# Twenty unread products before the first mask, and the second batch's keys turned two heads later

## The reference

```python
# attention: 2 batches, 8 heads, 576 rows, 64 columns a head
scores = q @ k.T / sqrt(64)
mask = scores >= (32nd largest score of the row)
attn = softmax(where(mask, scores, -1e9))
x = (attn @ v), heads side by side           # 1152 x 512
# mixture of 8 experts, all of them dense, F = 1024
P = exp(x @ w_gate - max), 8 rounds of row and column normalisation
x = sum over e of P[:, e] * (relu(x @ w1[e]) @ w2[e])
# last block, F = 2048
h = x @ w_in;  g = h * tanh(softplus(h));  out = g @ w_out
```

## Time and profile before

| | us |
|---|---|
| median of 3 executions | 1240.41 (1239.22 to 1242.2) |
| the profiled execution | 1242.88 |
| its span, first to last instruction | 1241.0 |
| PE busy | 1198.6 (97%) |
| DVE busy | 899.6 (72%) |
| ACT busy | 687.6 (55%) |
| POOL busy | 642.6 (52%) |

### The profile page before, as it was taken

One profiled execution on the slowest core, in us unless ns is written; L12 is line 12 of the kernel. 1 busy time (PEld: TensorE's weight loads), 2 busy tenths in 40 slices (PEclk: granted clock), 3 DMA queues, 4 the chain that ended last, 5 costly groups with the idle time before them and its releaser, 6 DMA issues.

```text
span 1241.0 us, 19573 instructions
## 1 busy us (share of the span) xinstructions
PE 1198.6 (97%) x6676; PEld 1071.3 (86%) x6676; DVE 899.6 (72%) x1556; ACT 687.6 (55%) x1226; POOL 642.6 (52%) x393
## 2 busy tenths in 40 slices
PE   4878999999999999999999999999999999999998
PEld 4777889999999998999888999999888888898777
DVE  6989998899999971446646564646464647887886
ACT  5666776767777664442243333333333337888776
POOL 1857965555656567763376666666666630000000
PEclk8599999999999999999999999999999999999999
DMA  9023432233323233332233222222222122222230
GB/s 170 9 86 120 144 104 93 94 94 107 110 90 111 86 111 102 120 102 93 85 106 107 69 75 76 75 80 74 86 67 94 52 68 85 69 69 84 86 125 36
DMA packets 150486, 112.10 MB, mean 90 GB/s; under 512 B 34832, under 2 KB 124944, under 8 KB 150416
## 3 DMA queue, kind: packets, MB, share of 16 engines
q1 hardware_dynamic: 150416, 111.19, 29.6%
HBM read 104.09 MB, written 7.08 MB: 90 GB/s over the span
## 4 chain that ended last, share of the span: by engine, by line
PE 86%; DVE 7%; ACT 3%; POOL 2%; issue 2%; DMA 1%; SPq 0%; ACTq 0%; DVEq 0%; POOLq 0%
PE ps L903 16%; PE ps L728 15%; PE ps L741 15%; PE ps L964 14%; PE ps L1031 7%; PE ps L1087 7%; PE ps L637 4%; PE ps L608 3%; DVE top L1486 2%; DVE work L1488 2%; PE ps L618 2%; PE ps L597 1%; POOL s_sb L1961 1%; PE ps L632 1%; POOL e_sb L1964 1%
## 5 line engine op out<-in xcount | busy, mean ns | idle before, releaser
L1890 POOL TENSOR_TENSOR w_lo<-w_raw,w_hi 128x1024 fp32r<-128x1024 f32 x90 | 219.6, 2440 | 114.4 <-ACT w_hi L1114 114.3
L1114 ACT ACTIVATE w_hi<-w_raw 128x1024 fp32r<-128x1024 f32 (+1 forms) x172 | 179.4, 1044 | 0.6 <-DMA w_raw<-in_k 0.6
L1486 DVE MAX8 top<-work 128x8 f32<-128x576 f32 x216 | 152.3, 747 | 0.0
L728 PE MATMUL ps<-x_hi,w_hi 128*128 128x384 f32 (+3 forms) x384 | 128.2, 334 | 0.1
L728 PE MATMUL ps<-x_hi,w_lo 128*128 128x384 f32 (+3 forms) x384 | 127.4, 332 | 0.0
L728 PE MATMUL ps<-x_lo,w_hi 128*128 128x384 f32 (+3 forms) x384 | 127.2, 331 | 0.0
L1897 POOL TENSOR_TENSOR ha_lo<-h_f,ha_hi 128x384 fp32r<-128x384 f32 (+1 forms) x72 | 72.0, 999 | 90.4 <-ACT ha_hi L1191 90.4
L903 PE MATMUL ps<-w_hi,h_lo 128*128 128x512 f32 x296 | 117.1, 396 | 0.0
L903 PE MATMUL ps<-w_lo,h_hi 128*128 128x512 f32 x296 | 116.9, 395 | 0.0
L903 PE MATMUL ps<-w_hi,h_hi 128*128 128x512 f32 x296 | 115.3, 390 | 0.0
L1488 DVE MATCH_REPLACE8 work<-top,work 128x576 f32<-128x576 f32 x144 | 105.9, 743 | 0.0
(11 more groups left out here) (185 smaller groups left out, 3273.1 us busy)
## 6 DMA issues: line engine op xcount, KB each, us to landing
w_raw<-in_moe_w SPq DMA_DIRECT2D x288, 256.0 KB, 3.0
w_raw<-in_moe_w_in SPq DMA_DIRECT2D x32, 256.0 KB, 2.8
w_raw<-in_moe_w_out SPq DMA_DIRECT2D x32, 256.0 KB, 3.1
spill<-y_out SPq DMA_DIRECT2D x5, 768.0 KB, 3.8
y_in<-spill SPq DMA_DIRECT2D x5, 768.0 KB, 4.4
q_parts<-in_q SPq DMA_DIRECT2D x18, 128.0 KB, 3.3
vones<-in_v SPq DMA_DIRECT2D x8, 256.0 KB, 4.9
out<-acc SPq DMA_DIRECT2D x8, 256.0 KB, 2.7
```

The lines of the kernel that those rows point to most:

```text
L728: last = nc.tensor.matmul(ps[:, bank, 0:w], wt[:, s, 0, c * P:(c + 1) * P], xt[:, c, token:token + w], start=(n == 0), stop=(n == len(term ...
L1114: return nc.scalar.activation(dst, src, ACT.Copy)
L1486: last = v_.max(top[:, b, op // 2, :], src)
L1890: g_.tensor_tensor(w_lo[:, s, :, :].rearrange("p a n -> p (a n)"), w_raw[:, s, :, :].rearrange("p a n -> p (a n)"), w_hi[:, s, :, :].rearr ...
```

## The change

TensorE's and ScalarE's programs of a tile turn and copy chunk `c` of the second batch's keys at the end of head `c + 3` instead of head `c + 1`: heads 3 to 7 of tile 1 instead of 1 to 5. Both waits inside are the same ones, counted from `c`. And TensorE issues twenty products of 128 x 512 into bank 7 (`X_BANK`), which nothing reads, in head 4 of tile 0: behind the waits for the queries' and keys' copies, ahead of the wait for the first mask.

```diff
+        KEYS_AT = 3
@@ TensorE, tile_body
                     if first and h == 4:
                         pe.wait_ge(q_copied, 4)
                         pe.wait_ge(k_copied, KEYS_0)
+                        keep_clock()
                     if late_parts is not None:
                         probs_transposed(late, (h - 4) % H)
...
-                    if keys and 1 <= h <= KC:
-                        pe.wait_ge(k_high, KC + h)
-                        pe.wait_ge(k_low1, h)
-                        if h == 1:
+                    if keys and KEYS_AT <= h < KEYS_AT + KC:
+                        c = h - KEYS_AT
+                        pe.wait_ge(k_high, KC + c + 1)
+                        pe.wait_ge(k_low1, c + 1)
+                        if c == 0:
                             pe.wait_ge(q_copied, 4)
                         else:
-                            pe.wait_ge(k_copied, KEYS_0 + 2 * h - 2)
-                        keys_transposed(1, h - 1, 0)
-                        keys_transposed(1, h - 1, 1)
+                            pe.wait_ge(k_copied, KEYS_0 + 2 * c)
+                        keys_transposed(1, c, 0)
+                        keys_transposed(1, c, 1)
+
+            def keep_clock():
+
+                for _ in range(20):
+                    nc.tensor.matmul(ps[:, X_BANK, :], q_s[:, 0, 0, :], k_s[:, 0, 0, 0:4 * P], start=True, stop=True)
@@ ScalarE, tile_body
-                    if keys and 1 <= h <= KC:
-                        keys_copied(1, h - 1, 0)
-                        keys_copied(1, h - 1, 1)
+                    if keys and KEYS_AT <= h < KEYS_AT + KC:
+                        keys_copied(1, h - KEYS_AT, 0)
+                        keys_copied(1, h - KEYS_AT, 1)
```

## The result

The change makes the kernel slower: median 1242.51 us (1238.91 to 1244.72, 18 executions) against 1240.51 us before (1239.22 to 1242.8, 18 executions), ratio 1.0015 with a 95% interval of 1.0008 to 1.0022. The forecast was 1238.1 us with a range up to 1241.5. A second series of the same kernel gave 1242.56 us against 1239.9 for the kernel before, ratio 1.0021 (1.0012 to 1.0030).

What follows compares the result with a forecast made beforehand. TensorE bounds the kernel from 130.7 us; ahead of it VectorE's search is the long string, with 4.64 us of stalls. Terms 2.2 + 0.5 - 0.6 = 2.1, taken as 2.3: 1240.41 - 2.3 = 1238.1 us, range 1235.4 to 1241.5.

Steps and rivals of the forecast that it cites:

- Part 1: Tile 1, heads 1 and 2: without key transposes, tile 0's row sums start 2.2 (high clock, 60%) or 0.6 us earlier.
- The sum: Gains and costs at 130 us: 2.2 + 0.5 - 0.6 = 2.1 us at high clock, 0.5 at low; 2.3 taken.
- both ends: Tile 0's last value products: clock high, gain 2.2 us (certain if transposes do not count as busy), or low, 0.6.
- Part 2: Tile 0, head 4: twenty products hold the clock up, making head 4 faster; +0.5 us taken, between -0.6 and +0.8.
- The case in between: Tile 0, head 4: clock falls at 26.7 us, twenty products end at 31.5, 1.4 late; later places about 0.6 later.
- rival (c): Tile 0: at low clock the twenty products hold TensorE until 33.8 us, delaying POOL's masks; slower, 1243.4 us; chance 8%.
- Part 3: Tile 1, heads 6 and 7: arriving keys delay scores (1,7) or the row sums; cost 0 to 1.4 us, 0.6 taken.
- The handing on to the end: From DVE's stall to 130 us: a DVE shift at 71 us reaches the end, except for the moved keys' cost.
- Rival (b): Tile 0's last value products run at low clock without the key transposes; gain 0.7 us, 1239.7 us; chance 22%.

## Why the prediction was wrong

**Part 1, the keys leave heads 1 and 2: this step failed.** Its sum was read from one execution in which TensorE was the late one, at the low clock from 47.3 to 64.2 us, so that 1.71 us of key transposes stood on the chain. In the second trace of before TensorE stands idle 1.50 and 1.12 us around the same transposes, they cost nothing, and the stall at the row sums is 0.30 instead of 3.81 us: what part 1 wanted to take out was not there. Measured, the term that was put at a gain of 2.2 or 0.6 us is a loss of 2.3 us (1.0021 twice). I named the other side of it, that the unbroken run which lets the clock rise gets shorter, and gave it 40% and a price of 1.6 us less gain; it was priced as a smaller gain where it is a loss. What the runs show in its place is both a rise that fails to come (two traces) and, which part 1 did not have, a fall of a clock that was up, in the longer waits (three traces). Whether the step holds in executions that go like the one I read stays open: the moved keys with six products at tile 2, in a trace whose clock was low as there until 43.6 us, had a span of 1238.6 against 1241.0, but the unmoved keys with the same six, in a trace as much alike, had 1238.4. I took one profiled execution, 2.5 us above the median of its kernel, as the place to work out a gain of 2 us.

**The sum.** Its own cases give 2.1 us with the clock high for the last value products and 0.5 with it low; at 60% for the first that is 1.5 us, 1238.9. I wrote 2.3, above the better of the two cases, for a reason (the profiled execution had the favourable case) that argues for less. That is an error of the sum beside that of the mechanism; without it the forecast would still have been a gain.

**The rule on transposes.** The Trainium skill says of the transpose mode, under "TensorE: Matmul & The Clock Gate", Part 4, that it does not count as busy for the clock in the same way as products do. The trace lists the transposes here as MATMUL with the identity and does not show whether they run in that mode. For these 32-bit ones the measurement decides, and it says that they do count: sixteen of them, unread, are the only difference between a kernel whose clock is low from 63.4 to 73.4 us and one in which it is up from 49.6 to 83.2, and between ratios of 1.0021 and 1.0001. I had kept both ends open; the trace's was right, and it was the end that speaks against the change.

**Part 2, the twenty products.** The case in between came true in both traces of the change: the clock fell at 26.3 and 26.4, the products took 6.4 us and ended at 32.3 and 31.8, against 31.5 worked out; they began at 26.1 and 25.6 instead of 25.3. After them the clock stayed high until 36.5, then fell before the first value products, as forecast. The term taken was +0.5 us, near the bound for products that run mostly at the high clock, where the case in between had been worked out at -0.6. Measured, the products alone are 0.5 us slower (0.04%, not told from nothing), so that the term was about 1 us too high, inside its bounds; rival (c) has the mechanism right (forty products: 4.0 to 4.7 us later) and the size wrong for twenty.

**Part 3, the keys arrive in heads 6 and 7.** Taken as 0.6 us. The traces of the change show neither a wait for the scores of (1,7) nor a longer one at tile 1's row sums (0.53 us, as before). With fuller heads the clock no longer fell at about 84 us: it does in all seven traces with unmoved keys (once from 75 to 85) and in one of the twelve with moved ones. With keys in place and sixteen transposes more, one trace has a wait of 0.70 us for (1,7) and the ratio is 1.0005; the moved keys with unread transposes have one of 0.32 us in their second trace. The term cannot be told from 0 nor from the 0.6 us that was taken.

**The handing on to the end.** That a shift of DVE at 71 us arrives at the end held in part: TensorE's wait for mask (2,3) at 128 us was not in my list, and in five of nine traces of kernels with moved keys and no products there the clock fell right behind it, for 3.4 us, which cost 1.2. Of the five such traces with unmoved keys one has it. Whether that share is due to the keys or to chance, so few traces do not tell; the six products there recovered 0.75 us.

**Rivals and chances.** Rival (b) had the place, the clock under tile 0's last value products, and gave 1239.7, a gain; it compared with a before that already was slow. The 7% for slower by over 0.2% was too little (the median itself, 0.15% and 0.21% above, lies at that border), since two of the three parts had a known way to a loss and the gain rested on a stretch that differs between executions.

## What to carry to other kernels

Work that lies in an engine's wait can be worth its place by what it does to the clock: before moving it, ask how long the waits become without it, and what runs right behind them. Where the granted clock goes up and down in the stretch of interest, one trace is one draw: take two or three of the same kernel before working out a gain of a few tenths of a per cent, and compare pairs of traces in which the clock went alike up to the edit. Unread work put in to hold the clock must end before what it waits for, at the low clock too: forty products that ended 4.0 us later cost 4.0 to 4.7 us.

## What the runs showed of the hardware

- One kernel's executions range over 3 to 6 us within a series (before: 1238.43 to 1244.86 in all series), and the traces show the low stretches of the clock at other places in each: before had them at 47.2 to 64.3 and 84.7 to 88.2 us in one trace, and at 83.9 to 87.1 alone (after 49.5) in another.
- The clock fell to 0.50 behind a stretch in which TensorE had been busy 7.95 of 13.40 us, with single waits of no more than 2.37 us (moved keys alone, 63.3 us).
- A low stretch of 3.4 us at about 131 us of this kernel costs 1.2 us at the end; one at 1043.4 us in the change's first trace costs nothing.
- Sixteen value products of 65 columns and 32 bits take 3.52 us at the low clock and 1.90 at the high one; at the low clock TensorE was busy with them and others for 15.57 of 16.90 us without the clock rising.
